# A banded attention stage: a third PSUM bank for the transposes of P, and the q and k tiles of the next pair turned one per unit

## The reference

```python
scores = scale * np.matmul(q, k.transpose(0, 1, 3, 2))
scores = np.where(keep, scores + bias, -1e9)
a = np.exp(scores - max); a = a / (sum(a) + 1e-9)
x = np.matmul(a, v)                          # to (B*S, H*D)
x = (h * np.tanh(softplus(h))) @ w_out       # h = x @ w_in
out = sum_e p[:, e] * (np.maximum(x @ w1[e], 0) @ w2[e])
```

## Time and profile before

| | |
|---|---|
| median of 3 runs | 897.05 us (896.2 to 897.34) |
| the profiled execution | 896.58 us, its span 894.6 us |
| TensorE matmul busy in the span | 866.6 us, 97% |
| VectorE, ScalarE, GpSimd busy | 491.7, 309.2, 260.9 us |
| TensorE busy, 50 to 75 us | 19.27 of 25 |
| TensorE busy, 100 to 125 us | 23.34 of 25 |
| TensorE busy, 175 to 500 us | all of it |
| TensorE's granted clock | full in the whole span |

### The profile page before, as it was taken

One profiled execution on the slowest core, in us unless ns is written; L12 is line 12 of the kernel. 1 busy time (PEld: TensorE's weight loads), 2 busy tenths in 40 slices (PEclk: granted clock), 3 DMA queues, 4 the chain that ended last, 5 costly groups with the idle time before them and its releaser, 6 DMA issues.

```text
span 894.6 us, 12640 instructions
## 1 busy us (share of the span) xinstructions
PE 866.6 (97%) x4918; PEld 438.7 (49%) x4918; DVE 491.7 (55%) x1016; ACT 309.2 (35%) x580; POOL 260.9 (29%) x222
## 2 busy tenths in 40 slices
PE   7878999999999999999999999999999999999998
PEld 6756776444444444444444444444444444444443
DVE  7878887999999999864432125222144321212121
ACT  5878875554554756541121010201010111101020
POOL 1646995222222222210049100086000392000000
PEclk9999999999999999999999999999999999999999
DMA  9961240000000000202000500002200000000001
GB/s 219 314 200 37 49 177 2 1 0 1 1 7 4 0 1 1 97 19 77 9 1 0 188 1 1 6 0 93 95 1 7 0 0 0 0 36 12 35 12 50
DMA packets 52005, 39.20 MB, mean 44 GB/s; under 512 B 40816, under 2 KB 41712, under 8 KB 51440
## 3 DMA queue, kind: packets, MB, share of 16 engines
q1 hardware_dynamic: 49888, 34.31, 12.7%
q10 hardware_dynamic: 2064, 4.19, 1.3%
HBM read 35.35 MB, written 3.15 MB: 43 GB/s over the span
## 4 chain that ended last, share of the span: by engine, by line
PE 87%; DVE 5%; ACT 5%; issue 2%; POOL 0%; DVEq 0%
PE bank L623 68%; PE bank L696 14%; ACT tmp L867 2%; PE bank L552 2%; ACT tmp L909 1%; PE bank L594 1%; PE bank L613 1%; DVE tmp L1145 1%; ACT scaled L883 1%; DVE wpieces L1094 1%; PE bank L571 1%; DVE xT L1254 1%; PE bank L507 1%; DVE tmp L1273 0%; ACT hid L860 0%
## 5 line engine op out<-in xcount | busy, mean ns | idle before, releaser
L978 ACT ACTIVATE hid<-bank 128x512 f16<-128x512 f32 x96 | 57.3, 597 | 422.2 <-PE bank L623 422.2
L623 PE MATMUL bank<-xT,wA 128*128 128x512 f16 (+1 forms) x864 | 194.6, 379 | 0.0
L1383 DVE SCALAR_TENSOR_TENSOR hid<-bank,hid 128x512 f16<-128x512 f32 x96 | 66.4, 692 | 181.7 <-ACT hid L978 181.7
L623 PEld LDWEIGHTS bank<-xT,wA 128*128 128x128 f16 x864 | 84.5, 98 | 100.6
L696 PE MATMUL bank<-hid,wB 128*128 128x512 f16 x576 | 132.1, 379 | 0.6 <-DVE xT L1254 0.6
L623 PE MATMUL bank<-xT,wB 128*128 x576 | 125.3, 379 | 0.0
L623 PE MATMUL bank<-wB,hid 128*128 128x512 f16 x576 | 125.3, 379 | 0.0
L623 PE MATMUL bank<-wA,hid 128*128 128x512 f16 x576 | 125.3, 379 | 0.0
L790 POOL TENSOR_SCALAR stage<-stage,sc 128x1024 f32<-128x1024 f32 x32 | 36.0, 1125 | 267.9 <-DVEq L1376 250.4
L833 POOL TENSOR_TENSOR tmp<-tmp 128x512 f32<-128x512 f32 x48 | 61.5, 1280 | 179.3 <-DVE tmp L1406 179.3
L1463 DVE SCALAR_TENSOR_TENSOR acc<-bank,pg,acc 128x512 f32<-128x512 f32 x36 | 27.0, 751 | 131.7 <-PE bank L623 131.7
(11 more groups left out here) (115 smaller groups left out, 930.5 us busy)
## 6 DMA issues: line engine op xcount, KB each, us to landing
stage<-in_moe_w SPq DMA_DIRECT2D x8, 2048.0 KB, 9.9
stage<-in_moe_w_in SPq DMA_DIRECT2D x1, 4096.0 KB, 14.4
wB<-in_moe_w_out ACTq DMA_DIRECT2D x1, 4096.0 KB, 16.6
hid<-in_q SPq DMA_DIRECT2D x16, 192.0 KB, 3.5
hid<-in_k SPq DMA_DIRECT2D x16, 192.0 KB, 3.5
xT<-in_v SPq DMA_DIRECT2D x8, 384.0 KB, 5.1
out_y<-acc SPq DMA_DIRECT2D x12, 256.0 KB, 2.0
rows<-max SPq DMA_DIRECT2D x4, 128.0 KB, 4.2
```

The costliest lines, as they stand in the source:

```text
L623: last = pe.matmul(dst, lhs(c, a), rhs(c, b), start=(c == 0 and n == 0), stop=(c == chunks - 1 and n == 2))
L978: act.activation(hv[:, f, 0, :], psum(f % 4), ACT.Relu).then_inc(f_hi, 1)
L1383: dve.scalar_tensor_tensor(hv[:, f, 1, :], psum(f % 4), 0.0, hv[:, f, 0, :], ALU.max, ALU.subtract).then_inc(f_ready, 1)
```

## The change

The third bank is bank 3 for every third unit in pairs 1 to 3 and in the first halves of pairs 4 to 6; elsewhere two banks are used as before. In pairs 1 to 6 each turn first transposes one tile of the next pair's q (even units) or k (odd units) into the last 128 columns of its own bank. ScalarE copies the q tile ahead of its copy of P, VectorE the k tile after its difference. The fills and their copies are left for pair 0 alone. The turn's waits include the tile of the bank's last user; the scores wait for the tiles that they use. `tr_psum` is raised at every third unit, so SP loads after unit 11 of a pair. The pieces of the weights stand at 22, 27, 32, 37 and 42, 47, 52, 57 (ScalarE) and 2 units later (VectorE), the maxima at 40 and 60, and the sharing at units 46 and 66 is done with the scores, in their bank; the scales are made at 45 and 65.

```diff
@@ -253,6 +253,7 @@
         tr_out = sem("tr_out")
+        tile_act, tile_dve = sem("tile_act"), sem("tile_dve")
         s_psum = sem("s_psum")
@@ -328,10 +329,10 @@
         BY_ACT, BY_DVE = range(PIECES // 2), range(PIECES // 2, PIECES)
-        W_ACT = [[start + gap * c for c in range(PIECES // 2)] for start, gap in ((2 * UNITS - 2, 4), (4 * UNITS - 8, 6))]
-        W_DVE = [[at + gap for at in units] for units, gap in zip(W_ACT, (2, 3))]
+        W_ACT = [[start + 5 * c for c in range(PIECES // 2)] for start in (2 * UNITS - 2, 4 * UNITS - 6)]
+        W_DVE = [[at + 2 for at in units] for units in W_ACT]
         W_MAX = ({n: units[-1] + 1 for n, units in enumerate(W_DVE)}, {0: UNITS + 8})
-        W_SHARE = ({n: at + 3 for n, at in W_MAX[0].items()}, {0: UNITS + 9})
+        W_SHARE = ({n: at + 6 for n, at in W_MAX[0].items()}, {0: UNITS + 9})
         W_FULL = [UNITS + c for c in range(PIECES // 2)]
@@ -374,12 +375,42 @@
-        def p_out(u, banded):
+        def p_bank(at):
+            m, u = divmod(at, UNITS)
+            two = m in (0, PAIRS - 1) or (m >= PAIRS - 4 and u >= UNITS // 2)
+            return 4 + u % 2 if two else (4, 5, 3)[u % 3]
+        def p_bank_before(at, this):
+            return max((n for n in range(at) if p_bank(n) == this), default=None)
+        def p_out(i, slot, u, banded):
             n = len(band[u // 2]) * P
-            return psum(4 + u % 2, n), pT_b[u % 3][:, :, 0:n]
+            return psum(p_bank((2 * i + slot) * UNITS + u), n), pT_b[u % 3][:, :, 0:n]
+        def tile_at(at):
+            m, u = divmod(at, UNITS)
+            return (u % 2, u // 2, (m + 1) % 2) if 1 <= m < PAIRS - 1 else None
+        def tile_on_dve(at):
+            return at % 2 == 1
+        def tile_psum(at):
+            return psum(p_bank(at), P, 3 * P)
+        def tiles_out(at):
+            tiles = [n for n in range(UNITS, at + 1) if tile_at(n)]
+            on_dve = sum(tile_on_dve(n) for n in tiles)
+            return len(tiles) - on_dve, on_dve
@@ -500,9 +531,6 @@
                     pe.wait_ge(tr_out, FILLS * m + k)
-                if banded and k == 0 and isinstance(m, int):
-                    if m >= PAIRS - 2:
-                        pe.wait_ge(x_ready, m - PAIRS + 3)
                 for n, t in enumerate(tiles):
@@ -522,6 +550,9 @@
                         pe.wait_ge(tr_out, 2 if u == 0 else FILLS)
+                elif banded and 2 * i + slot >= 2:
+                    if u % 2 == 0:
+                        wait_tiles((2 * i + slot - 1) * UNITS + u + 1)
                 elif u == 0:
@@ -539,6 +570,14 @@
+            def wait_tiles(at):
+                by_act, by_dve = tiles_out(at)
+                if by_act:
+                    pe.wait_ge(tile_act, by_act)
+                if by_dve:
+                    pe.wait_ge(tile_dve, by_dve)
             def scores(i, slot, u, banded):
@@ -552,6 +591,9 @@
                             last.then_inc(s_psum, 1)
+                for n, unit in W_SHARE[0].items():
+                    if (2 * i + slot) * UNITS + u == unit:
+                        share_max(n, psum(u % 3, P, 3 * P))
@@ -576,20 +618,37 @@
+            def wait_split(at):
+                pe.wait_ge(pT_act, at + 1)
+                pe.wait_ge(pT_dve, at + 1)
+                wait_tiles(at)
             def turn(i, slot, u, banded):
                 src = s_b[u % 3] if banded else s_g
-                dst, _ = p_out(u, banded)
+                dst, _ = p_out(i, slot, u, banded)
                 at = UNITS * (2 * i + slot) + u
-                if banded and at >= 2:
-                    pe.wait_ge(pT_act, at - 1)
-                    pe.wait_ge(pT_dve, at - 1)
                 if banded:
-                    for n, unit in W_SHARE[0].items():
-                        if at == unit:
-                            share_max(n, psum(4 + u % 2, P, 3 * P))
+                    used = p_bank_before(at, p_bank(at))
+                    if used is not None:
+                        wait_split(used)
+                    elif p_bank(at) == 3:
+                        pe.wait_ge(tr_out, FILLS * 2)
+                        pe.wait_ge(v_scale, 2)
+                    turned = sum(n < at for n in X0_BANDED)
+                    if p_bank(at) == 3 and turned:
+                        pe.wait_ge(x_ready, turned)
+                    tile = tile_at(at)
+                    if tile:
+                        j, t, to = tile
+                        if u == 0:
+                            pe.wait_ge(qk_loaded[to], 64 * ((2 * i + slot + 1) // 2 + 1))
+                        moved = pe.transpose(tile_psum(at), nat[to][j][:, t * P:(t + 1) * P], ident[:])
+                        if u % 3 == 2:
+                            moved.then_inc(tr_psum, 1)
                 for b in range(len((band if banded else full)[u // 2])):
@@ -605,7 +664,7 @@
                     pe.wait_ge(o_ready, 2 * m + 1 + u // (UNITS // 2))
-                _, pt = p_out(u, banded)
+                _, pt = p_out(i, slot, u, banded)
                 keys = [kt for kt, _ in (band if banded else full)[qt]]
@@ -653,7 +712,7 @@
                         pv(i, slot, u, banded)
-                    if after(i, slot) and u in FILL_AT:
+                    if after(i, slot) and u in FILL_AT and (not banded or before(i, slot) is None):
                         fill(*after(i, slot), FILL_AT.index(u), banded)
@@ -661,7 +720,10 @@
                             pe.wait_ge(x_ready, c)
-                        pe.wait_ge(tr_out, FILLS * min(2 * i + slot + 2, PAIRS))
+                        if banded:
+                            wait_split(p_bank_before((2 * i + slot) * UNITS + u + 1, 3))
+                        else:
+                            pe.wait_ge(tr_out, FILLS * min(2 * i + slot + 2, PAIRS))
                         turn_x(0, c)
@@ -860,6 +922,19 @@
+            def copy_tile(at):
+                if not tile_at(at) or tile_on_dve(at):
+                    return
+                j, t, to = tile_at(at)
+                if j == 0:
+                    m = at // UNITS + 1
+                    last = act.activation(qT_sb[to][:, t * P:(t + 1) * P], tile_psum(at), ACT.Copy,
+                                          scale=q_scale[:, m:m + 1])
+                else:
+                    last = act.copy(kT_sb[to][:, t * P:(t + 1) * P], tile_psum(at))
+                last.then_inc(tile_act, 1)
             def expo(i, slot, u, banded):
@@ -905,12 +980,14 @@
                     act.wait_ge(pT_psum, PB * i + UNITS * slot + u + 1)
-                    src, pt = p_out(u, banded)
+                    if banded:
+                        copy_tile((2 * i + slot) * UNITS + u)
+                    src, pt = p_out(i, slot, u, banded)
                     act.activation(pt[:, 0], src, ACT.Copy, scale=P_SCALE).then_inc(pT_act, 1)
                         expo(*ahead, banded)
-                    if following and u - 1 in FILL_AT:
+                    if following and u - 1 in FILL_AT and (not banded or before(i, slot) is None):
                         copy_out(*following, FILL_AT.index(u - 1))
@@ -1141,6 +1218,9 @@
                     dve.wait_ge(s_psum, UNITS * m + u + 1)
+                    for n, unit in W_SHARE[0].items():
+                        if UNITS * m + u == unit:
+                            matrix_max(n, psum(u % 3, P, 3 * P))
                     dve.sem_inc(carrier, 1)
@@ -1212,7 +1292,7 @@
                         weights_max(n)
-                    if banded and at == W_SHARE[0][n] + 1:
+                    if banded and at == W_SHARE[0][n] - 1:
                         matrix_scale(n)
@@ -1265,12 +1345,12 @@
                     dve.wait_ge(pT_act, base + u + 1)
-                    if banded:
-                        for n, unit in W_SHARE[0].items():
-                            if (2 * i + slot) * UNITS + u == unit:
-                                matrix_max(n, psum(4 + u % 2, P, 3 * P))
-                    src, pt = p_out(u, banded)
+                    src, pt = p_out(i, slot, u, banded)
                     dve.scalar_tensor_tensor(pt[:, 1], src, P_SCALE, pt[:, 0], ALU.mult, ALU.subtract).then_inc(pT_dve, 1)
+                    at = (2 * i + slot) * UNITS + u
+                    if banded and tile_at(at) and tile_on_dve(at):
+                        _, t, to = tile_at(at)
+                        dve.tensor_copy(kT_sb[to][:, t * P:(t + 1) * P], tile_psum(at)).then_inc(tile_dve, 1)
                     if meanwhile:
```

## The result

The changed kernel took 904.91 us (median of 6; 903.04 to 905.58), the kernel before 897.06 beside it: ratio 1.0082, interval 1.0067 to 1.0097. The forecast was 897.7 in a range of 892.8 to 902.0; slower had 0.29. The profiled execution took 905.03 us, its span 903.1, at a mean granted clock of 0.991 where the profiled one before had 1.000.

What follows compares the result with a forecast made beforehand. It took a ring of waits between VectorE and ScalarE to bound pairs 2 to 4, TensorE pair 1. The ledger's +0.6 us on the profiled 896.58 gave 897.2, plus 0.47 for the median 897.7; range 892.8 to 902.0.

Steps and rivals of the forecast that it cites:

- The ring as the bound of pairs 2 to 4: Attention pairs: VectorE's difference and biased scores and ScalarE's exponential and copy of P wait for each other, setting the length.
- The third bank at no price: Transposes of P: a third bank mostly renames TensorE's wait; bounds 0 and -1.6 us, taken as 0.
- Pairs 1, 5 and 6 as TensorE's, with the tiles at nothing or less: Pair 1: TensorE the bound, 0; pair 5: -0.8 us of wait, at most to TensorE's time; pair 6: hidden in idle, 0.
- the ledger: Sum of changes per pair, VectorE's in pairs 2 to 4: 0, -0.7, +1.1, +1.9, -1.7, 0; together +0.6 us.
- A copy of k, 0.21 us, 1.3 a pair: VectorE's six new k tile copies per pair: 0.21 us each between bounds 0.21 and 0.29, 1.3 us per pair.
- ScalarE's total stays, in smaller blocks: ScalarE's six q tile copies per pair, 2.1 us, take about the time of its four old q and k copies.
- Pieces at 0.9 us each: Weight pieces moved between pairs: pair 2 -0.9, pair 3 +0.9, pair 4 +1.2, pair 5 -1.2 us.
- Pair 5 down to TensorE's 14.22: Pair 5 loses a piece (-1.2) and a wait (-0.8), at most to TensorE's 14.22 of 15.89 us: -1.7.
- GpSimd's chain: Splits of w_in and w_out: the scale comes 6.0 us later with 6.7 allowed; just not the bound, idle near 0.
- Rival B: Slower: VectorE's k copies in the ring cost their whole duration; +5.1 us, 902.2; chance 0.23.
- the sign of it that I named: Pairs 1 or 6 over 14.5 us would show B.

Runs made afterwards that it cites:

- e6: Kernel before with each of the 16 weight pieces cut from 1024 to 64 columns; 888.14 us.
- e4: Changed kernel with two banks for the transposes of P throughout, no third bank; 904.50 us.
- e1: Changed kernel with the weight pieces back at the units of the kernel before; 899.81 us.
- e16: Changed kernel with weight pieces cut to 64 columns and VectorE's copies of the k tiles left out; 893.17 us.
- e14: Changed kernel with weight pieces cut to 64 columns and the tile copies on both ScalarE and VectorE left out; 889.25 us.
- e12: Kernel before with the new units of the weight pieces, plus eight short fp16 products at places where TensorE waits behind a piece; 900.84 us.
- e5: Changed kernel with each of the 16 weight pieces cut from 1024 to 64 columns; 894.42 us.
- e15: Changed kernel with short fp16 products where TensorE waits behind a weight piece and also ahead of turns 58 to 61 and 63; 903.71 us.
- e17: Changed kernel with ScalarE's pieces at the old units, VectorE's first four at the same units, its second four 3 units behind; 900.14 us.
- e11: Changed kernel with eight short fp16 products at the 14 or so places where TensorE waits behind a weight piece; 903.17 us.
- e2: Kernel before with nothing but the new units of the weight pieces, maxima shared at units 44 and 65; 901.83 us.
- e13: Kernel before with VectorE's first four weight pieces at ScalarE's units, its second four 3 units behind as before; 893.22 us.

## Why the prediction was wrong, point by point

- **The ring as the bound of pairs 2 to 4:** right (without pieces pair 2 falls from 18.14 to 13.63, e6). **The third bank at no price:** right (e4).
- **Pairs 1, 5 and 6 as TensorE's, with the tiles at nothing or less:** the step that failed for the tiles. With the pieces at the old units (e1, all at full clock) the tiles cost 1.8 us in pairs 2 to 4, where the ledger had 1.2, but 0.7, 1.1 and 0.8 in pairs 1, 5 and 6, where it had 0, -0.8 and 0. Those pairs hung on the ring too.
- **A copy of k, 0.21 us, 1.3 a pair:** right in duration; in effect 2.7 us over six pairs (e16), less than the 0.2 x 36 = 7.2 of the rows. The rest must be hidden in idle time; no run shows where.
- **"ScalarE's total stays, in smaller blocks", priced at nothing:** wrong. ScalarE's busy time was the same, yet ahead of each second copy of P there is now 0.36 us in the ring, 4.4 us in all (e16, e14). The old large copies together cost about 1.7 over six pairs (e6, e14), while the ledger credited 2.7 to their end in pairs 2 to 4 alone. I counted totals and not what stands between a transpose and its release.
- **Pieces at 0.9 us each:** wrong size, by place. One VectorE piece more in pair 4, with the closer spacing, cost 2.9 us at full clock (15.96 to 18.83, e12), one ScalarE piece fewer in pair 2 gave 0.3, one more in pair 3 cost 1.1, and the piece that left pair 5 gave 0.5 (15.89 to 15.39), not 1.2. Without tiles the new units cost 3.2 us at full clock, where the ledger had 0.
- **Pair 5 down to TensorE's 14.22:** the largest miss of one pair, 14.2 against 18.55. Even without pieces and tiles it takes 15.44 (e6), with tiles 16.50 (e5); the clock adds 2.1. A busy time of one engine is a bound, not a forecast.
- **The clock:** not considered. In the profile before it was 1.00 in every window of the stage, and I took that as fixed. 3.0 of 9.8 us in the profiled execution.
- **GpSimd's chain:** the scale did come later and the chain was no bound, as the ledger had it, but by luck of the longer stage: the idle time is 6.50 us and not near 0.
- **Rival B** had the sign, and the sign of it that I named came true: pairs 1 and 6 are over 14.5. Its mechanism did not: it put 7.8 us on the k copies, which took 2.7, and had nothing on ScalarE's q copies or the clock. That 902.2 comes within 2.7 us is in part luck.

Of the 9.8 us of the profiled pairs, where the ledger had 0.6: tiles 4.4 (e1), clock 3.0 (e15), units of the pieces the remaining 2.4, or 3.2 as e12 has them without tiles. Since e17 shows that the causes do not simply add, this split holds for these placements only.

## What to carry to other kernels

Where two engines pass work around a ring, price an added instruction by what waits between it and the ring's next step, not by the engine's idle total, and do so in every iteration, also where the matrix engine looks like the bound. When both must do side work, try it at the same moment; here it gained without the tiles and not with them. Before moving stalls about, look at what is left of the matrix engine's work there: waits of 1.1 to 1.2 us one behind the other were followed by the lower clock, and the matrix work behind them paid. A few large copies split into many small ones, at equal busy time of ScalarE and with half of them new on VectorE, cost several microseconds.

## What the runs showed of the hardware

- Two waits of TensorE, 1.07 and 1.19 us with 0.7 us of work between them, stood ahead of a granted clock of 1.2 GHz in the middle of the stage; it fell within the third, of 1.06 us. In pair 5 some 9.6 us at 1.2 GHz (e11) cost 2.7 us against none (e15); in pair 2 of e2, 3.3 us at 1.2 GHz cost 0.3, and the ring was the bound there.
- A VectorE product of one column took 1.00 us (before) and 1.11 (e15) beside a GpSimd tensor product and 0.15 (after, e13) without it. Moving the end of a stage by a microsecond or two turns this on and off.
